# An own order of steps for each engine in a chunked recurrence, with the state grown in PSUM

## The reference

```python
for t in range(S):
    y[:, :, t] = np.einsum('bhd,bhde->bhe', rt, state)
    Sa = np.einsum('bhde,bhe->bhd', state, at)
    state_decay = state * wt[:, :, None, :] - np.einsum('bhd,bhe->bhde', Sa, bt)
    state = state_decay + np.einsum('bhd,bhe->bhde', vt, kt)
x = y as (3072, 320)
x = (1 / (1 + exp(-(x @ w_gate))) * (x @ w_val)) @ w_out      # 320 -> 1536 -> 320
out = max(x @ w1, x @ w2, x @ w3) @ w_out2                    # 320 -> 768 -> 320
```

## Time and profile before

| | us |
|---|---|
| median of 3 executions | 1123.53 (1121.59 to 1126.89) |
| the profiled execution, its time | 1123.35 |
| its span, first to last instruction | 1121.6 |
| granted TensorE clock, mean over the span | 0.954 of 2.4 GHz |
| last `y_t` of the recurrence begins | 443.13 |

### The profile page before, as it was taken

The page is one execution under the profiler, slowest core; times in us unless marked ns, Lnnn a source line. Parts: engine busy times, 40 slices in busy tenths (PEclk is TensorE's granted clock), DMA queues, the critical chain, the costliest instruction groups (busy, mean ns, idle before and its releaser), DMA issues. The chain is left out here.

```text
span 1121.6 us, 21667 instructions
## 1 busy us (share of the span) xinstructions
PE 1039.6 (93%) x8872; PEld 867.0 (77%) x8872; DVE 514.6 (46%) x875; ACT 352.0 (31%) x732; POOL 291.3 (26%) x527
## 2 busy tenths in 40 slices
PE   6577999899989996999999999999997999999998
PEld 3445778787778885788888888888885888888886
DVE  6726776567774443553323223332225543342432
ACT  3213544444444442432222222222223211111111
POOL 4788869588785500000000000000000000000000
PEclk7766999899999998899999999999998999999999
DMA  7632345455522225630000200000002100000000
GB/s 173 157 78 68 94 112 136 95 135 131 125 71 71 72 65 136 177 97 0 29 1 23 60 1 1 1 0 0 0 0 64 45 24 23 1 24 8 16 23 23
DMA packets 53247, 66.23 MB, mean 59 GB/s; under 512 B 19944, under 2 KB 40680, under 8 KB 53160
## 3 DMA queue, kind: packets, MB, share of 16 engines
q1 hardware_dynamic: 53160, 65.00, 22.7%
HBM read 57.12 MB, written 7.86 MB: 58 GB/s over the span
## 5 line engine op out<-in xcount | busy, mean ns | idle before, releaser
L1144 DVE TENSOR_TENSOR hid<-gate,gbank 128x512 f32<-128x512 f32 x72 | 49.5, 688 | 204.1 <-ACT gate L1090 204.1
L875 PE MATMUL mbank<-x_hi,w_hi 128*128 128x512 f32 x324 | 127.7, 394 | 6.7 <-DVE w_lo L1329 6.7
L392 POOL TENSOR_TENSOR inv_step<-lab 128x30 f32<-128x30 f32 (+9 forms) x180 | 120.0, 667 | 35.9 <-DVE lab L682 22.2
L875 PE MATMUL mbank<-x_hi,w_lo 128*128 128x512 f32 x324 | 127.0, 392 | 0.0
L1090 ACT ACTIVATE gate<-gbank 128x512 f32<-128x512 f32 x72 | 43.1, 598 | 226.4 <-PE gbank L875 226.4
L400 POOL TENSOR_TENSOR lab<-lab,inv_step 128x30 f32<-128x30 f32 (+9 forms) x180 | 110.4, 613 | 14.1
L1346 DVE TENSOR_TENSOR hid<-hid,mbank 128x512 f32<-128x512 f32 x72 | 49.5, 687 | 97.3 <-PE mbank L875 94.2
L875 PE MATMUL gbank<-x_hi,g_hi 128*128 128x512 f32 x216 | 84.9, 393 | 8.0 <-DVE v_lo L1124 8.0
L875 PE MATMUL mbank<-x_lo,w_hi 128*128 128x512 f32 x216 | 85.3, 395 | 0.0
L1045 PE MATMUL gbank<-h_hi,o_hi 128*128 128x512 f32 x216 | 84.1, 390 | 1.0 <-DVE h_lo L1150 1.0
L875 PE MATMUL gbank<-x_hi,g_lo 128*128 128x512 f32 x216 | 84.8, 392 | 0.0
(11 more groups left out here) (130 smaller groups left out, 2015.0 us busy)
## 6 DMA issues: line engine op xcount, KB each, us to landing
lent_w<-kb_in SPq DMA_DIRECT2D x12, 720.0 KB, 6.7
r_m<-rm_in SPq DMA_DIRECT2D x24, 360.0 KB, 3.7
lent_x<-w_in SPq DMA_DIRECT2D x10, 742.5 KB, 6.1
a_t<-a_in SPq DMA_DIRECT2D x12, 360.0 KB, 4.7
r_t<-r_in SPq DMA_DIRECT2D x11, 360.0 KB, 6.6
vu_rows<-v_in SPq DMA_DIRECT2D x24, 160.0 KB, 6.1
out<-o_sb SPq DMA_DIRECT2D x6, 640.0 KB, 3.2
x<-y_t SPq DMA_DIRECT2D x48, 60.0 KB, 3.2
```

Source lines behind the costliest of these rows:

```text
L392: product = nc.gpsimd.tensor_tensor(part, column, row, op=ALU.mult)
L875: last = mm(out, w, x, start=n == 0, stop=n == len(seq) - 1)
L1144: nc.vector.tensor_tensor(hid[:, m % 2, :], gate[:, m % 2, :], p_val[m % 2][:, :], op=ALU.mult).then_inc(hid_done, 1)
```

## The change

- Each engine has its own list of steps (`TURN[engine]`), and for the lead-in up to the end of pair 0 one explicit list (`LEAD[engine]`) of step, pair and part. Turns now run from 0 (the lead-in) to 13.
- `inc` no longer multiplies the state by the identity. VectorE adds the old state to `p_ds` in PSUM and multiplies the sum by `decay_mask`, both for four slots in one instruction. ScalarE makes `decay_mask` from the block mask and decay (step `dm`, four instructions a group).
- `ga` and `gr` take the banks `p_ga` and `p_gr` in turn, in TensorE's order of gram units.
- All copies of u (four a group) are ScalarE's.
- `lab_rows` of unit 5 is copied by ScalarE, of units 0 to 4 by GpSimd.
- Neighbouring `t1`, `low` and `t2` steps of different groups are issued head by head, mixed (`chain`).
- In the lead-in GpSimd does `scale_a` and `scale_kb` of pair 1; SyncE loads kb ahead of a, and other loads in another order. `keep_warm` in the first solve comes every 6 steps of the solve from the 6th (before: every 3 from the 24th).
- The solve stays on GpSimd, with the same instructions; the first one has its own semaphore.

```diff
+TURN = {
+    "PE": """
+    vx.0 ty.2 ga.0 ga.1 vt.0 ga.2 ga.3 kb.0 ga.4 ga.5 ts.0 vx.1 ts.1 t1.0 gr.0 gr.1 t1.1 low.0 vt.1 vx.2 gr.2 y.0
+    low.1 t2.0 kb.1 gr.3 t1.2 t2.1 ty.0 vt.2 inc.0 kb.2 low.2 y.1 gr.4 gr.5 ty.1 inc.1 t2.2 ts.2 y.2 inc.2
+    """,
+    "DVE": """
+    mask_a.0 mask_a.1 mask_a.2 mask_a.3 mask_a.4 mask_a.5 scale_y.2 lab.0 scan.0 mask_r.0 mask_r.1 scan.1 decay.0
+    mask_r.2 mask_r.3 scale_y.0 scale_a.0 next.0 scale_kb.0 scale_y.1 mask_r.4 mask_r.5 next.1 scale_kb.1 next.2
+    inv.0
+    """,
+    "ACT": """
+    b.0 am.2 vu.0 dm.0 kb.0 lab.5 state.0 b.1 u1.0 state.1 vu.1 b.2 low.0 u1.1 y.0 low.1 kb.1 u2.0 u1.2 vu.2 dm.1
+    kb.2 low.2 y.1 u2.1 dm.2 u2.2 am.0 y.2 am.1 state.2
+    """,
+    "POOL": """
+    lab.0 lab.1 lab.2 lab.3 lab.4 solve.0
+    """,
 }
+LEAD = {
+    "PE": """
+    kb.0.0 ga.0.0 ga.0.1 ga.0.2 ga.0.3 ga.0.4 ga.0.5 ga.1.0 ga.1.1 ga.1.2 ga.1.3 ga.1.4 ga.1.5 kb.0.1 kb.0.2 kb.1.0
+    kb.1.1 kb.1.2 vx.0.0 ga.2.0 kb.2.0 ga.2.1 kb.2.1 vx.0.1 ga.2.2 ga.2.3 ga.2.4 ga.2.5 kb.2.2 ga.3.0 ga.3.1 ga.3.2
+    ga.3.3 ga.3.4 ga.3.5 t1.0.0 t1.0.1 kb.3.0 kb.3.1 low.0.0 low.0.1 vx.0.2 t1.0.2 kb.3.2 low.0.2 t2.0.0 inc.0.0
+    t2.0.1 inc.0.1 t2.0.2 inc.0.2
+    """,
+    "DVE": """
+    scan.0.0 scan.0.1 decay.0.0 scale_kb.0.0 scale_a.0.0 scale_kb.0.1 scan.1.0 mask_a.0.0 scan.1.1 mask_a.0.1
+    decay.1.0 mask_a.0.2 mask_a.0.3 mask_a.0.4 scan.2.0 mask_a.0.5 mask_a.1.0 mask_a.1.1 mask_a.1.2 mask_a.1.3
+    mask_a.1.4 mask_a.1.5 lab.0.0 scan.2.1 decay.2.0 scale_a.2.0 scale_kb.2.0 scale_kb.2.1 scan.3.0 mask_a.2.0
+    scan.3.1 mask_a.2.1 scale_kb.3.0 decay.3.0 mask_a.2.2 scale_a.3.0 mask_a.2.3 scan.4.0 scale_kb.3.1 mask_a.2.4
+    scan.4.1 mask_a.2.5 mask_a.3.0 decay.4.0 mask_a.3.1 scale_kb.4.0 mask_a.3.2 scale_a.4.0 mask_a.3.3 mask_a.3.4
+    inv.0.0 mask_a.3.5 lab.2.0 next.0.0 next.0.1 next.0.2 scale_kb.4.1
+    """,
...
+    "POOL": """
+    lab.0.0 scale_kb.1.0 lab.0.1 scale_a.1.0 scale_kb.1.1 lab.0.2 lab.0.3 lab.0.4 lab.1.0 lab.1.1 lab.1.2 lab.1.3
+    lab.1.4 solve.0.0 lab.2.0 lab.2.1 lab.2.2 lab.2.3 lab.2.4 lab.3.0 lab.3.1 lab.3.2 lab.3.3 lab.3.4 solve.2.0
+    """,
+}
@@
             load_w(0)
+            load_kb(0)
             load_a(0)
-            load_kb(0)
             load_w(1)
+            load_kb(1)
             load_a(1)
-            load_kb(1)
             load_w(2)
+            load_kb(2)
             load_a(2)
-            load_kb(2)
-            for k in range(2):
-                load_v(k)
+            load_v(0)
+            load_kb(3)
+            load_a(3)
+            load_rm(0, 0)
             load_w(3)
-            load_a(3)
-            load_kb(3)
+            load_v(1)
+            load_w(4)
+            load_kb(4)
+            load_a(4)
+            load_rm(0, 1)
             load_r(1)
-            load_rm(0, 0)
-            load_rm(0, 1)
-            load_w(4)
-            load_a(4)
-            load_kb(4)
             load_v(2)
@@ def increment
                 pe.wait_ge(s_done, n)
-                if k > 0:
-                    mm(p_ds[0:hd, 0:4 * hd], ident[0:hd, 0:hd], s_t[0:hd, 4 * g:4 * g + 4, 0:hd],
-                       start=True, stop=False, skip_group_check=True)
-                pe.wait_ge(u2_kept[0], n + 1)
-                pe.wait_ge(u2_kept[1], n + 1)
+                pe.wait_ge(u2_kept, n + 1)
@@ def gram_bank_free
+                use = GRAM_USE[name, k, u]
+                if use >= 2:
+                    before, kb, ub = GRAMS[use - 2]
+                    pe.wait_ge(akm_done if before == "ga" else grm_done, 6 * kb + ub + 1)
@@ def next_state
-                for at in range(4):
-                    s = 4 * g + at
-                    last = nc.vector.scalar_tensor_tensor(
-                        s_t[0:hd, s, 0:hd], p_ds[0:hd, at * hd:at * hd + hd], decay[0:hd, k % 4, s:s + 1],
-                        diag_mask[0:hd, :, :].rearrange("e i d -> e (i d)")[:, 0:hd], op0=ALU.mult, op1=ALU.mult)
-                last.then_inc(s_done, 1)
+                nc.vector.tensor_tensor(new, new, state, op=ALU.add).then_inc(grown, 1)
+                dve.wait_ge(grown, n + 1)
+                dve.wait_ge(dm_done, n + 1)
+                nc.vector.tensor_tensor(state, new, decay_mask[0:hd, n % 2, :, 0:hd], op=ALU.mult).then_inc(s_done, 1)
@@ ScalarE, def keep_u1 (keep_u2 in the same way)
-                copy(vu_rows[64:96, k % 3, 1, GO[g]:GO[g] + GW[g]],
-                     chain_bank(g, 1)[64:96, 0:GW[g]]).then_inc(u1_kept[1], 1)
+                for par in (1, 0):
+                    at = 64 * par
+                    last = copy(vu_rows[at:at + C, k % 3, par, GO[g]:GO[g] + GW[g]],
+                                chain_bank(g, par)[at:at + C, 0:GW[g]])
+                last.then_inc(u1_kept, 1)
@@ ScalarE, new
+            def mask_decay(k, g):
+                n, hd = 3 * k + g, HD[g]
+                if n >= 2:
+                    act.wait_ge(s_done, n - 1)
...
+                for at in range(4):
+                    s = 4 * g + at
+                    last = copy(decay_mask[0:hd, n % 2, at, 0:hd], mask, decay[0:hd, k % 4, s:s + 1])
+                last.then_inc(dm_done, 1)
@@ TensorE, new: mixed t1, low, t2
+                for h in range(2 * HPS[0]):
+                    for par in (1, 0):
+                        if first is not None and h < 2 * HPS[first]:
+                            last_first = solve_first(k, first, h, par)
+                        if low is not None and h < 2 * HPS[low]:
+                            last_low = lower(k, low, h, par)
+                        if second is not None and h < 2 * HPS[second]:
+                            last_second = solve_second(k, second, h, par)
```

More of the change, by code:

```diff
@@ L72 @@
-PAIR_OF = {"vx": 0, "t1": 0, "low": 0, "t2": 0, "inc": 0, "ts": 0, "vt": -1, "gr": -1, "y": -1, "ty": -1,
-           "ga": 3, "kb": 3, "scan": 4, "decay": 4, "scale_a": 4, "scale_kb": 4}
-def steps(turn):
-    for name, x in (TURN if turn >= 0 else LEAD_IN[turn]):
-        if name == "am":
-            k = turn + (3 if x == 2 else 4)
-        elif name == "lab":
-            if turn % 2:
-                continue
-            k = turn + 2
-        elif name == "inv":
-            if not turn % 2:
-                continue
-            k = turn + 1
-        elif name == "ty" and x == 2:
-            k = turn - 2
-        else:
-            k = turn + PAIR_OF[name]
-        if not 0 <= k < PAIRS:
+TURN = {
[15 more added lines that the diff above has]
+    """,
+}
@@ new lines, with steps @@
+PAIR_OF = {"PE": {"vt": -1, "gr": -1, "y": -1, "ty": -1, "ga": 3, "kb": 3},
+           "DVE": {"mask_r": -1, "scale_y": -1, "mask_a": 3, "scan": 4, "decay": 4, "scale_a": 4, "scale_kb": 4,
+                   "lab": 2, "inv": 1},
+           "ACT": {"vu": -1, "y": -1, "kb": 3, "lab": 3, "am": 4},
+           "POOL": {"lab": 3, "solve": 2}}
+EVEN, ODD = ("DVE lab", "POOL solve"), ("DVE inv",)
+def steps(engine, turn):
+    if turn == 0:
+        for word in LEAD[engine].split():
+            name, k, x = word.split(".")
+            yield name, int(k), int(x)
+        return
+    for word in TURN[engine].split():
+        name, x = word.split(".")
+        k, x = turn + PAIR_OF[engine].get(name, 0), int(x)
+        if (name, x) in (("ty", 2), ("scale_y", 2), ("am", 2)):
+            k -= 1
+        if turn % 2 and f"{engine} {name}" in EVEN or not turn % 2 and f"{engine} {name}" in ODD:
@@ L94, in steps @@
             continue
-        if name == "ts" and k == 0 or name == "inc" and k == PAIRS - 1:
+        if not 0 <= k < PAIRS or name in ("inc", "next", "dm") and k == PAIRS - 1:
             continue
         yield name, k, x
-TURNS = range(FIRST, PAIRS + 2)
-TR_USE = {}
+TURNS = range(PAIRS + 2)
+CHAIN = ("t1", "low", "t2")
+TR_USE, GRAM_USE = {}, {}
 for _turn in TURNS:
-    for _name, _k, _x in steps(_turn):
+    for _name, _k, _x in steps("PE", _turn):
         if _name in ("ts", "vt", "kb"):
@@ L106 @@
             TR_USE[_name, _k, _x] = len(TR_USE)
+        elif _name in ("ga", "gr"):
+            GRAM_USE[_name, _k, _x] = len(GRAM_USE)
+GRAMS = tuple(GRAM_USE)
+LAB_ACT = (5,)
+LAB_POOL = tuple(u for u in range(6) if u not in LAB_ACT)
+BY_POOL = (1,)
 def since(value):
```

339 lines of the change are left out of this document (194 added, 145 removed), and 10 rows, old and new, of tables (LEAD_IN, TURN).

## The result

The median of the changed kernel is 1092.75 us (four runs, 1091.52 to 1094.04), of the kernel before 1123.93 (1121.59 to 1126.89). Their ratio is 0.9721, 95% interval 0.9695 to 0.9748: 31 us less, where 28 were forecast. The profiled executions took 1093.35 and 1123.35 us, with spans of 1091.6 and 1121.6, so 30.0 us are to be explained.

The account below looks back on a forecast made before the run. Bound by GpSimd's solve loop and TensorE's work in the recurrence, 63.5 us per two turns with misfit. Gains of 4 (start), 18 (loops), 5 (last turns) and 1 (banks) sum to 28: 1123.35 - 28 = 1095 us, range 1083 to 1114.

Parts of the forecast that it names:

- The loops: Second to fifth inverse: three loops of two turns each take 57.5 us instead of 63.5, 18 us gained.
- The solve loop: GpSimd's loop between inverses: solve 44.9, lab copies 8.6, lab transpose 1.9 and 0.3 more, 55.7 us.
- the misfit: Time lost per loop to steps in an order that suits not all engines: about 5 us, of which 2 stay.
- an unforced turn of TensorE: TensorE's work in a full turn of the kernel before, nearly without gaps: 29.4 us, 58.8 for two.
- mixing: Interleaving t1, low and t2 on TensorE: counted as 0, with 1.0 us a turn as upper end.
- The product: Identity product on TensorE, removed by the change: 2.4 us in each of turns 1 to 10.
- The second inverse: Inverse after the second solve: comes when that solve ends, at 136.5 us against 140.5, 4 us gained.
- The last part: Last turns, bound by TensorE: 5 us gained, and 1 us for the last turn's gram banks.
- A, the loop stays near 62: Rival: denser VectorE work or blocking keeps the solve loop near 62 us, only 14.5 us gained, 1109; chance 0.13.
- B, the clock: Rival: TensorE rests before inverses, lower clock costs 3.5 us in each of four even turns, total 1109; chance 0.09.
- C, ScalarE in the chain: Rival: ScalarE's added 6.4 us a turn delays the chain: 1163 in full, chance 0.06; 1128 if half, 0.08.
- D, the mixing is empty: Rival: the change does less than it says; interleaving t1, low and t2 gains nothing; no chance given.

Follow-up runs that it names:

- Experiment 2: Changed kernel with 15 of the 30 steps of each solve, inverse left incomplete: 1075.59 us in a single run, loops of 52.2 us.
- Experiment 5: Changed kernel with 28 instead of 40 warming matmuls in the first solve: 1094.92 us; then also with reordered lead-in lists of ScalarE and TensorE: 1087.94 us.
- experiments 1: Changed kernel with the identity product issued again before each group's increment and overwritten, as work only: 1102.88 us, ratio 0.9785 to the kernel before.
- experiment 6: Changed kernel with t1, low and t2 issued one after the other, not mixed: 1094.41 us; the same with the reordered start: 1089.9 us.
- experiment 8: Changed kernel with half of the copies of u back on VectorE: 1098.32 us, ratio 0.9754 to the kernel before.
- experiment 3: Kernel before with all parts of the change except the engines' own orders, the mixing and the new start: 1114.21 us, ratio 0.989.
- the reordered start: Changed kernel with other lead-in lists for ScalarE and TensorE and 28 instead of 40 warming matmuls: 1087.94 us, ratio 0.9672 to the kernel before.

## Why the prediction was right, and where it was wrong

**The loops: right in kind, 7 us too careful.** The solve loop was put at 44.9 + 8.6 + 1.9 + 0.3 = 55.7 us. The one from the third inverse is 55.55: 8.13 from inverse to lab, 1.96 of transpose, 45.5 of solve, with the clock dip in it; the next has no dip and takes 55.60. The 20 copies take 7.52 us (196.88 to 204.40), not 8.6: 10.30 x 20/24 was too high a price. The step that failed is the misfit: "In-order queues never fit fully; of the 5 us of misfit I keep 2". 57.5 stood in the sum, 55.1 was measured; lab transposes were to come 11 us behind inverses and come 7.5 behind them. Experiment 2 says why none is left: TensorE needs 52.2 us, 3 fewer than GpSimd, not 1.7 fewer as the forecast's 54.0 had it. Two terms made that: an unforced turn of TensorE was overrated (27.9 with the product back and mixing, so 28.6 without mixing if the two add up, against 29.4), and mixing was set to 0 and is 0.7 us a turn (1.0 was its upper end). The product was overrated the other way, 2.4 for 1.9; why it costs less than its records say is not shown.

**The second inverse: wrong.** Each term of the start held: first inverse 86.5 (86), second solve from 96.1 (96), 39.6 us long (39.9), end 135.6 (136.5). The step that failed is the silent one, that the inverse comes when its solve ends. The forecast costed the lead-in by GpSimd alone and never followed pair 0 through ScalarE's new list. In the earlier trace rows the inverse at 140.54 had waited 2.97 us for GpSimd, so VectorE stood ready at 137.6. Now it gets there at 142.78, 5.2 us later: that eats the reserve of 3 us, loses 2.2, and leaves unused that the solve ends 5 us sooner. Experiment 5 shows where the time goes: other lists for ScalarE and TensorE give 5.0 us back, and with fewer warm matmuls 6.5, by which the inverse follows its solve. kb and a of pair 2 were issued at 39.16 and 39.52, not near 34; the first inverse, for which VectorE waited 5.90 us, covered it.

**The last part: right in sum.** 6.0 us were forecast and came. The late turns went from 23.9 to 22.15 us where 21.5 was named. Product and mixing together would make 2.55 less by experiments 1 and 6, and 1.75 came: the own orders, or ScalarE's part in them, seem to give 0.8 a late turn back. Of that 0.3 is visible as idle time of TensorE (0.9 us in 22.15, with a wait of 0.7 for vu_t, against 0.6 in 23.9). This was not tried alone. That the sum came out is in part luck again: the clock is low for 6.8 us behind the fifth inverse of the changed kernel, and for 4 us at the end of the kernel before.

**The state step, the copies, the masks.** Two instructions of 667 and 658 ns replace 1.34 us by 1.33 (1.39 forecast, PSUM written at no extra price). Four decay masks take 1.25 us, 1.12 for the narrow group: 3.6 a turn as forecast. ScalarE is busy 21.84 of 27 us (20), VectorE 20.59 (20.8). The copies of u were put at 0 with 2.2 as upper end; experiment 8 makes it 0 or a gain.

**The rivals.** A, the loop stays near 62, did not come, but is what experiment 3 measures: the loop stays near 62 if the shared order stays. B, the clock: in the turns it falls for 3.4 us behind the third inverse and for 6.8 behind the fifth, 1.7 and 3.4 us of TensorE's time. The first falls into a loop in which GpSimd binds by 3 us, and moves the lab transpose by 0.5. The second is not covered: with the reordered start no dip falls behind the fifth inverse, and the state product that the changed kernel reaches at 389.33, 81.3 us behind that inverse, comes 2.7 us sooner behind its own (380.29 - 301.64 = 78.65). And the forecast left the clock out where it is low for longest: from 98 to 118.5 pair 0 runs at the lower level, 20.5 us against 17 in the kernel before. C, ScalarE in the chain: it counted in the lead-in only, as part of 5.0 us, and not in the turns, where 5 us of ScalarE are idle. D, the mixing is empty: a turn gains 0.7 us from it, though the total shows no gain (experiment 6); the row of 18 ns a record spoke for an overlap that was there already, and there was more of it to be had, 10 ns a record mixed. The floor of about 25 ns that the Trainium skill gives (TensorE: Matmul & The Clock Gate, Part 1) does not hold in this trace.
